# Rows of 520 instead of 512 columns for the x tiles and the h slots of an experts stage

## The chip, the cores and the metric

The kernel runs on one core of one Trainium2 chip, as one program. The metric is the device time of that core in microseconds (us), from the program's start to its end. Lower is better.

## The reference, cut to what matters

The first part is a gated linear attention with a recurrent state. Its output goes through a bilinear layer, and the result `x` (3072 tokens by 384) through four experts whose outputs are added with gate weights. The change is in the experts:

```
def _moe2_ref(x, domain_probs, w1, w2):        # x: 3072 x 384, w1: 4 x 384 x 1024, w2: 4 x 1024 x 384
    E = w1.shape[0]
    p = domain_probs / (domain_probs.sum(-1, keepdims=True) + 1e-09)
    out = np.zeros((N, D), dtype=np.float32)
    for e in range(E):
        h = np.maximum(x @ w1[e], 0.0)
        out += p[:, e:e + 1] * (h @ w2[e])
    return out
```

## The kernel before, in words

All work is in float32. Where a product is large, each operand is split into a high part (rounded to the type fp32r) and the low rest, and one product is made of three: high by high, high by low and low by high (`TERMS` is 3). TensorE therefore has three matmuls where the formula has one.

**Stages.** From 0 to about 414 us of the profiled span, TensorE folds two weight matrices (`w3` and `w_out`) into one, then works on the attention (six chunks of 128 steps in each of four batches) and beside it on the bilinear layer: for each batch two tiles of 384 tokens and eight blocks of 128 features, with `up1` (18 matmuls of 384 columns: line 1022, 1023 and 1024 are its three terms) and `down1` (9 of 384 columns, same lines). The visits to the attention ("visit", lines 1031 to 1084) are short bursts of small matmuls between them. The bilinear layer writes x, high and low part apart, to two DRAM tensors.

**The experts**, from about 414 us to the end, are the stage of the change. The work is four experts `e`, three rounds `m` of each, and 16 steps `s` of a round. A round has two tiles of x of `TILE2` = 512 tokens, tile `u = s // 8`; a step takes block `f = s % 8` of 128 features of h:

- `up2_product` (line 1175) makes h of the step: 9 matmuls of 512 columns, with a 128x128 block of the first weight matrix of the expert as the stationary operand and 512 columns of the x tile as the moving one. `k` is the block of 128 rows of x (three), and the terms are in this order: `we_hi` by `x_hi`, `we_hi` by `x_lo`, `we_lo` by `x_hi`. These are called **up** matmuls below.
- ScalarE writes `h_hi` = relu of the PSUM bank (line 601), VectorE then `h_lo` = relu of the bank minus `h_hi` (line 821). Both have two slots, `s % 2`.
- `down2_product` (line 1294) makes the expert's output: 12 matmuls of 384 columns, with 128 columns of `h_hi` or `h_lo` as the stationary operand and 384 columns of the second weight matrix as the moving one (terms: `h_hi` by `we_hi`, `h_hi` by `we_lo`, `h_lo` by `we_hi`). These are called **down** matmuls below. VectorE adds the sums to `total` with the gate (line 1000).

`step2` writes the order of the two by hand: the 12 down matmuls of step s with the 9 up matmuls of step s + 2 set between them, so that the pattern of seven matmuls "down, down, up, down, up, down, up" runs three times in a step:

```
for i in range(SUBS * TERMS):
    down2_product(e, m, s, i)
    if ahead and i % SUBS >= 1:
        up2_product(ahead[0], ahead[2], ups)
        ups += 1
```

Every matmul has a weight load of its own (the engine row PEld): while one matmul streams its moving operand out of SBUF, the stationary operand of the next one is read out of SBUF too. A pair "A, then B" below is matmul A streaming while B's stationary operand is loaded.

**Loads.** SyncE's queue brings each x tile (high and low part, 768 KB each) into one of two slots (`load_x1`) when the tile that was there has been used up, 24 times in all, and the weights of the next expert once an expert.

**Where the tiles lie.** A partition's tensors lie one after another in the order in which `sb(...)` makes them, each rounded up to 32 bytes. Counted modulo 512 bytes of the partition's address: `h_hi` and `h_lo` start at 480, as do all of the expert's weight tensors (`we_hi`, `we_lo`, both slots), the weights of the bilinear layer (`wb_hi`, `wb_lo`, `wp_hi`, `wp_lo`) and their moving operands (`x0`, `g_hi`, `g_lo`). The four x tiles of the experts (`x1_0_hi`, `x1_0_lo`, `x1_1_hi`, `x1_1_lo`) start at 192. Every row of 512 columns is 2048 bytes and every row of 384 columns 1536 bytes, and every 128 columns are 512 bytes, so that all blocks of a tensor lie at the same address modulo 512 as its start. The distance of a pair is the address of the moving operand minus that of the stationary one that is loaded beside it, modulo 512. Before the change it has two values in the experts: 224 for up, then down (and up, then up), and 0 for down, then down, and for down, then up.

Of the kernel before, what the change touches and what calls it, by code (L numbers as in the profile page):

```python
# [24 lines left out]
F32 = mybir.dt.float32  # L25
F32R = mybir.dt.float32r
ALU = mybir.AluOpType
ACT = mybir.ActivationFunctionType
AX = mybir.AxisListType

P = 128
# [12 lines left out]
KT, FT = DM // P, FF // P  # L44
# [9 lines left out]
TILE2 = 512  # L54
TILES2 = TOKENS // TILE2
SUBS = TILE2 // P
STEPS2 = 2 * FT
ROUNDS = TILES2 // 2
WSET = 2 * KT * FF
PIECE = 512  # L60
# [21 lines left out]
BY_TENSOR = STATES - 1  # L82

ATTENTION_COLUMNS = (SLOTS * 3 + 2 + 2 + 2 + 1) * PAIRS * CHUNK + SLOTS * VD + PAIRS * P + PAIRS * D + PAIRS * ODD + 2 * PAIRS
ATTENTION_REST = ATTENTION_COLUMNS - 4 * KT * TILE2
REDO_X0 = 2 * CHUNKS


def gated_attention_experts(nc, akq, v, akq_long, v_columns, w3T, w_out, wsets, probs, out):
    x1_dram = [nc.dram_tensor(f"x1_{part}_spill", [P, KT, TOKENS], F32, kind="Internal").ap() for part in ("hi", "lo")]  # L90
# [3 lines left out]
    with ExitStack() as ctx:  # L94
        def sb(name, shape, dt=F32, where=ctx):
            return where.enter_context(nc.sbuf_tensor(name, shape, dt))

        def sem(name):
            return ctx.enter_context(nc.semaphore(name))

        bank = [ctx.enter_context(nc.psum_tensor(f"bank{i}", [P, 512], F32)) for i in range(5)]
# [8 lines left out]
        gate = sb("gate", [P, TOKENS // P, EXPERTS])  # L110
        gate_sum = sb("gate_sum", [P, TOKENS // P])
        gate_inv = sb("gate_inv", [P, TOKENS // P])
        h_hi = sb("h_hi", [P, 2, TILE2], F32R)
        h_lo = sb("h_lo", [P, 2, TILE2], F32R)
        outside = sb("outside", [PD, BATCH * CHUNKS])
        outside_sum = sb("outside_sum", [1, 1])
        regular = sb("regular", [1, 1], mybir.dt.int32)
# [49 lines left out]
        we_raw, we_hi, we_lo, x1_hi, x1_lo = [None, None], [None, None], [None, None], [None, None], [None, None]  # L167
# [6 lines left out]


        for slot in range(2):
            x1_hi[slot] = sb(f"x1_{slot}_hi", [P, KT, TILE2], F32R)
            x1_lo[slot] = sb(f"x1_{slot}_lo", [P, KT, TILE2], F32R)
        sb("attention_rest", [P, ATTENTION_REST])
        we_hi[1] = sb("we1_hi", [P, WSET], F32R)  # L180
        raw = ExitStack()
# [84 lines left out]
        x1_loaded = [sem(f"x1_loaded{i}") for i in range(2)]  # L266
        up_done = sem("up_done")
        h_hi_ready = sem("h_hi_ready")
        h_lo_ready = sem("h_lo_ready")
# [49 lines left out]
        def _(sp):  # L319
# [47 lines left out]

            def load_x1(n):
                slot, at = n % 2, n % TILES2 * TILE2
                sp.dma_start(x1_hi[slot][:, :, :].bitcast(F32), x1_dram[0][:, :, at:at + TILE2]).then_inc(x1_loaded[slot], 16)  # L370
                sp.dma_start(x1_lo[slot][:, :, :].bitcast(F32), x1_dram[1][:, :, at:at + TILE2]).then_inc(x1_loaded[slot], 16)

            def load_w3(k):
                sp.dma_start(w3_sb[:, k, 0:FOLD_FIRST * P], w3T[:, k, 0:FOLD_FIRST * P]).then_inc(w3_loaded[k], 16)
# [73 lines left out]
            with sp.If(is_regular == 1):  # L448
                load_x1(0)
                load_x1(1)  # L450
# [3 lines left out]
            with sp.If(is_regular == 0):  # L454
                with sp.Fori(0, BATCH) as b:
                    for t in range(TILES1):
                        store_x1(BATCH + b, t, b * SEQ + t * TILE1)
                sp.wait_ge(x1_stored, X1_AHEAD + 32 * TILES1 * 2 * BATCH)
                load_x1(0)
                load_x1(1)  # L460
            sp.sem_inc(x1_final, 1)
            for e in range(EXPERTS):
# [4 lines left out]
                for tile in range(TILES2):  # L467
# [4 lines left out]
                    if e + 1 == EXPERTS:  # L472
                        count = 1 if tile + 1 == TILES2 else SUBS
                        for i in range(0, SUBS, count):
                            sp.wait_ge(added, ADDED_AHEAD + SUBS * n + i + count)
                            at = slice(tile * SUBS + i, tile * SUBS + i + count)
# [71 lines left out]
        def _(act):  # L548
# [49 lines left out]

            def h_high(n, s):
                act.wait_ge(up_done, STEPS2 * n + s + 1)  # L600
                act.activation(h_hi[:, s % 2, :], bank[s % 2][:, :], ACT.Relu).then_inc(h_hi_ready, 1)  # L601

            def bilinear(b, beside=True, last_batch=False):
                for s in range(STEPS1):
# [75 lines left out]
            with act.If(is_regular == 0):  # L680
                with act.Fori(0, BATCH) as b:
# [26 lines left out]
                    g_high(BATCH + b, 0)  # L708
                    bilinear(BATCH + b, beside=False)
                h_high(0, 0)  # L710


            def round_high(e, m, last):
                for s in range(STEPS2):
                    if s + 1 < STEPS2 or not last:
                        h_high(e * ROUNDS + m, s + 1)
                    if e + 1 < EXPERTS and s % FT == 4:
                        act.wait_ge(x1_final, 1)
                        pieces_high(2 + e, 2 * m + s // FT)

            for e in range(EXPERTS):
                last_expert = e == EXPERTS - 1
                with act.Fori(0, ROUNDS - last_expert) as m:
                    round_high(e, m, False)
            round_high(EXPERTS - 1, ROUNDS - 1, True)


        @block.vector
        def _(dve):
# [88 lines left out]

            def h_low(n, s):
                dve.wait_ge(h_hi_ready, STEPS2 * n + s + 1)  # L820
                dve.scalar_tensor_tensor(out=h_lo[:, s % 2, :], in0=bank[s % 2][:, :], scalar=0.0,  # L821
                                         in1=h_hi[:, s % 2, :], op0=ALU.max, op1=ALU.subtract).then_inc(h_lo_ready, 1)

            def piece_low(i):
                at = slice(i * PIECE, (i + 1) * PIECE)
# [26 lines left out]
            def bilinear(b, beside=True, last_batch=False):  # L852
                for s in range(STEPS1):
# [24 lines left out]
                    if last_batch and beside and s == STEPS1 - 1:  # L878
                        with dve.If(flag == 1):
                            h_low(0, 0)  # L880
# [122 lines left out]
            def round_low(e, m, last):  # L1003
                for s in range(STEPS2):
                    if s + 1 < STEPS2 or not last:
                        h_low(e * ROUNDS + m, s + 1)
                    if s % FT == FT - 1:
                        add(e, m, s // FT)
# [3 lines left out]
            for e in range(EXPERTS):  # L1012
                with dve.Fori(0, ROUNDS - (e == EXPERTS - 1)) as m:
                    round_low(e, m, False)
            round_low(EXPERTS - 1, ROUNDS - 1, True)


        @block.tensor
        def _(pe):
            def split_product(dst, left, right, first, last):  # L1020

                pe.matmul(dst, left[0], right[0], start=first, stop=False)  # L1022
                pe.matmul(dst, left[0], right[1], start=False, stop=False)  # L1023
                return pe.matmul(dst, left[1], right[0], start=False, stop=last)  # L1024
# [145 lines left out]
            def up2_product(e, s, i):  # L1170

                u, f = divmod(s, FT)
                k, term = divmod(i, TERMS)
                cols = slice(k * FF + f * P, k * FF + (f + 1) * P)
                mm = pe.matmul(bank[s % 2][:, :], (we_hi if term < 2 else we_lo)[e % 2][:, cols], (x1_lo if term == 1 else x1_hi)[u][:, k, :],  # L1175
                               start=(i == 0), stop=(i == KT * TERMS - 1))
                if i == KT * TERMS - 1:
                    mm.then_inc(up_done, 1)

            def up2(e, m, s):  # L1180
                up2_waits(e, m, s)
                for i in range(KT * TERMS):
                    up2_product(e, s, i)
# [31 lines left out]
            for k in range(FT):  # L1215
# [5 lines left out]
                for f in range(FOLD_FIRST):  # L1221
                    if (k, f) == (0, 1):
                        pe.wait_ge(w3_loaded[0], 16)
                    cols = slice(f * P, (f + 1) * P)
                    if k < SPLIT_FROM:
                        mm = pe.matmul(bank[FOLD_BANKS[f]][:, 0:DM], w3_sb[:, k, cols], wo_sb[:, k, :], start=(k == 0), stop=False)  # L1226
                    else:
                        i = k - SPLIT_FROM
                        mm = split_product(bank[FOLD_BANKS[f]][:, 0:DM], (w3_hi[:, i, cols], w3_lo[:, k, cols]),
                                           (wo_hi[:, i, :], wo_lo[:, i, :]), False, k == FT - 1)  # L1230
# [7 lines left out]
            for n in range((FT - FOLD_FIRST) * FT):  # L1238
                f, k = FOLD_FIRST + n // FT, n % FT
# [4 lines left out]
                mm = pe.matmul(bank[FOLD_BANKS[f]][:, 0:DM], w3_sb[:, k, f * P:(f + 1) * P], wo_sb[:, k, :], start=(k == 0), stop=(k == FT - 1))  # L1244
# [14 lines left out]
            with nc.body("redo_products", valid_engines=[pe.engine]):  # L1259
                with pe.Fori(0, BATCH) as b:  # L1260
                    with pe.Fori(0, REDO_ROWS) as i:
                        pe.wait_ge(redo_product_ready, REDO_ROWS * b + i + 1)
                        for c in range(CHUNKS):
                            mm = pe.matmul(bank[5][:, 2 * c:2 * c + 2], redo_product[:, c * CHUNK:(c + 1) * CHUNK], head_sum[:, :],
                                           start=True, stop=True)
                        mm.then_inc(redo_summed, 1)
                    for c in range(CHUNKS):
# [3 lines left out]
                        for k in range(KT):  # L1271
                            mm = pe.transpose(bank[7][:, k * P:(k + 1) * P], y_sb[:, k * P:(k + 1) * P], identity[:, :])
# [26 lines left out]
            def step2(e, m, s, ahead):  # L1299

                pe.wait_ge(h_lo_ready, STEPS2 * (e * ROUNDS + m) + s + 1)
                if ahead:
                    up2_waits(*ahead)
                ups = 0
# [5 lines that stand above are left out]
# [72 lines left out]
```

## Time and profile before

| | |
|---|---|
| runs | 1219.95 us median of 3 (1218.94 to 1220.34) |
| profiled execution, span of its instructions | 1217.6 us |
| TensorE busy (matmul) | 1212.3 us, 100% of the span, 7740 matmuls |
| TensorE weight loads busy | 1118.6 us, 92%, 7740 loads |
| VectorE / ScalarE / GpSimd busy | 461.4 / 281.7 / 168.8 us |
| granted TensorE clock | 1.000 of full speed |
| DMA | 108.03 MB, mean 89 GB/s |

The profile is of one execution, whose instructions span 1217.6 us; what lies around the span makes up the rest to the measured time. The busy time of a matmul in it overlaps the next one's (matmuls are pipelined, their ends are modelled), so the time that a matmul takes from the engine is read from the distance between two starts in the timeline, not from its busy time. The timeline prints starts to 0.01 us; over ten or more matmuls that is better than 1 ns each.

### The profile page before, as it was taken

To read this page: it belongs to the slowest core of one execution; us is meant where nothing else is said; L and a number is where in the kernel's file an instruction comes from. 1 tells how busy PE (TensorE), PEld (TensorE's weight loads), DVE (VectorE), ACT (ScalarE), POOL (GpSimd) and SP (SyncE) were. 2 spreads that over 40 slices of the span, in tenths; PEclk is the share of its full clock that TensorE was granted. 3 is DMA by queue.
4 is the path that set the end of the run, shared out by engine and by line. 5 is a ranking of instruction groups with operands and counts; after the bars stand their busy time and mean duration, and the time that the engine had idled before them with its cause. 6 is when DMAs were issued, how large, how long until landed. Compare 5 with 4: busy or idle time off the path is not lost.

```text
span 1217.6 us, 18865 instructions
## 1 busy us (share of the span) xinstructions
PE 1212.3 (100%) x7740; PEld 1118.6 (92%) x7740; DVE 461.4 (38%) x886; ACT 281.7 (23%) x526; POOL 168.8 (14%) x148
## 2 busy tenths in 40 slices
PE   9999999999999999999999999999999999999998
PEld 8799999999999999999999999999999999999998
DVE  6997586586651122122222222222122222222222
ACT  3443333333333311111111111111111111111111
POOL 1132222222223520000000000000000000000000
PEclk9999999999999999999999999999999999999999
DMA  9644444544415331100141111123101111222201
GB/s 286 207 121 122 126 132 106 137 128 105 126 47 195 106 145 52 51 17 36 53 156 52 52 52 52 52 73 135 42 15 46 52 52 53 78 78 78 78 9 44
DMA packets 87543, 108.03 MB, mean 89 GB/s; under 512 B 38576, under 2 KB 57904, under 8 KB 86960
## 3 DMA queue, kind: packets, MB, share of 16 engines
q1 hardware_dynamic: 87184, 106.63, 28.0%
q8 instruction: 52, 0.85, 0.3%
q10 hardware_dynamic: 288, 0.39, 0.1%
q14 instruction: 19, 0.16, 0.0%
HBM read 86.29 MB, written 18.35 MB: 86 GB/s over the span
## 4 chain that ended last, share of the span: by engine, by line
PE 99%; DVE 0%; issue 0%; DVEq 0%; ACT 0%
PE bank L1175 33%; PE bank L1294 25%; PE bank L1022 9%; PE bank L1024 9%; PE bank L1023 9%; PE score_banks L1294 8%; PE bank L1063 2%; PE bank L1244 1%; PE score_banks L1084 1%; PE bank L1073 1%; PE score_banks L1047 1%; PE bank L1226 1%; PE bank L1214 0%; DVE total L1000 0%; PE bank L1031 0%
## 5 line engine op out<-in xcount | busy, mean ns | idle before, releaser
L821 DVE SCALAR_TENSOR_TENSOR h_lo<-bank,h_hi 128x512 fp32r<-128x512 f32 x192 | 132.8, 691 | 584.9 <-ACT h_hi L601 584.0
L601 ACT ACTIVATE h_hi<-bank 128x512 fp32r<-128x512 f32 x192 | 114.7, 597 | 661.7 <-PE bank L1175 661.7
L1175 PE MATMUL bank<-x_hi,we_lo 128*128 128x512 f32 x576 | 228.7, 397 | 0.0
L1175 PE MATMUL bank<-x_hi,we_hi 128*128 128x512 f32 x576 | 224.1, 389 | 0.0
L1175 PE MATMUL bank<-x_lo,we_hi 128*128 128x512 f32 x576 | 223.5, 388 | 0.0
L1294 PE MATMUL bank<-we_hi,h_hi 128*128 128x384 f32 x576 | 194.6, 338 | 0.0
L1294 PE MATMUL bank<-we_lo,h_hi 128*128 128x384 f32 x576 | 194.5, 338 | 0.0
L1294 PE MATMUL bank<-we_hi,h_lo 128*128 128x384 f32 x576 | 193.8, 336 | 0.0
L499 POOL TENSOR_TENSOR we_lo<-we_raw,we_hi (+1 forms) x48 | 60.9, 1289 | 527.8 <-ACT we_hi L562 527.8
L1175 PEld LDWEIGHTS bank<-x_hi,we_lo 128*128 128x128 f32 x576 | 108.3, 188 | 22.4
L1175 PEld LDWEIGHTS bank<-x_lo,we_hi 128*128 128x128 f32 x576 | 108.0, 188 | 22.7
L1022 PE MATMUL bank<-x,wb_hi 128*128 128x384 f32 x384 | 128.6, 335 | 0.0
L1024 PE MATMUL bank<-x,wb_lo 128*128 128x384 f32 x384 | 128.3, 334 | 0.0
L1023 PE MATMUL bank<-x,wb_hi 128*128 128x384 f32 x384 | 128.3, 334 | 0.0
L1294 PEld LDWEIGHTS bank<-we_hi,h_hi 128*128 128x128 f32 x576 | 108.3, 188 | 8.5
L1294 PEld LDWEIGHTS bank<-we_hi,h_lo 128*128 128x128 f32 x576 | 108.3, 188 | 8.4
L1175 PEld LDWEIGHTS bank<-x_hi,we_hi 128*128 128x128 f32 x576 | 108.3, 188 | 0.2
L1294 PEld LDWEIGHTS bank<-we_lo,h_hi 128*128 128x128 f32 x576 | 108.1, 188 | 0.0
L510 POOL TENSOR_TENSOR g_lo<-g_sb,g_hi 128x384 fp32r<-128x384 f32 x64 | 66.3, 1036 | 221.3 <-ACT g_hi L591 221.3
L811 DVE TENSOR_TENSOR g_sb<-a_sb,bank 128x384 f32<-128x384 f32 x64 | 35.3, 552 | 110.8 <-PE bank L1024 110.8
L1022 PEld LDWEIGHTS bank<-x,wb_hi 128*128 128x128 f32 x384 | 72.1, 188 | 0.2 <-issue 0.2
L1023 PEld LDWEIGHTS bank<-x,wb_hi 128*128 128x128 f32 x384 | 72.1, 188 | 0.1
(99 smaller groups left out, 1473.3 us busy)
## 6 DMA issues: line engine op xcount, KB each, us to landing
x_hi<-x_hi_spill SPq DMA_DIRECT2D x24, 768.0 KB, 4.8
x_lo<-x_lo_spill SPq DMA_DIRECT2D x24, 768.0 KB, 6.3
we_raw<-wset SPq DMA_DIRECT2D x4, 3072.0 KB, 10.0
inputs<-akq SPq DMA_DIRECT2D x24, 448.0 KB, 5.2
values<-v_rows SPq DMA_DIRECT2D x24, 256.0 KB, 3.7
inputs<-akq SPq DMA_DIRECT2D x24, 224.0 KB, 3.3
x_hi_spill<-x_hi_out SPq DMA_DIRECT2D x8, 576.0 KB, 4.3
x_lo_spill<-x_lo_out SPq DMA_DIRECT2D x8, 576.0 KB, 5.2
```

The lines of the kernel that those rows point to most:

```text
L499: pool.tensor_tensor(set_lo(n)[:, at], set_raw(n)[:, at], set_hi(n)[:, at], ALU.subtract).then_inc(piece_lo, 1)
L510: pool.tensor_tensor(g_lo[:, s % 2, :], g_sb[:, s % 2, :], g_hi[:, s % 2, :], ALU.subtract).then_inc(g_lo_ready, 1)
L601: act.activation(h_hi[:, s % 2, :], bank[s % 2][:, :], ACT.Relu).then_inc(h_hi_ready, 1)
L811: dve.tensor_tensor(g_sb[:, s % 2, :], a_sb[:, s % 2, :], bank[1][:, 0:TILE1], ALU.mult).then_inc(g_ready, 1)
L821: dve.scalar_tensor_tensor(out=h_lo[:, s % 2, :], in0=bank[s % 2][:, :], scalar=0.0, in1=h_hi[:, s % 2, :], op0=ALU.max, op1=ALU.subtract) ...
L1022: pe.matmul(dst, left[0], right[0], start=first, stop=False)
L1023: pe.matmul(dst, left[0], right[1], start=False, stop=False)
L1024: return pe.matmul(dst, left[1], right[0], start=False, stop=last)
L1047: mm = pe.matmul(bank[5 + half][rows, STATE_AT + i * D:STATE_AT + (i + 1) * D], keys_t[:, pair, rows], values[:, c % SLOTS, at], start=(i ...
L1063: mm = pe.matmul(bank[7][q * ODD:(q + 1) * ODD, (2 * row + g) * CHUNK:(2 * row + g + 1) * CHUNK], values[:, c % SLOTS, at], scores[:, row, ...
L1175: mm = pe.matmul(bank[s % 2][:, :], (we_hi if term < 2 else we_lo)[e % 2][:, cols], (x1_lo if term == 1 else x1_hi)[u][:, k, :], start=(i ...
L1294: mm = pe.matmul(bank[SUM_BANKS[sub]][:, 0:DM], (h_hi if term < 2 else h_lo)[:, s % 2, rows], (we_lo if term == 1 else we_hi)[e % 2][:, cols],
```

## The change

Each row of an x tile and each slot of h becomes 520 columns (2080 bytes) long, of which the first 512 are used as before. `h_rest` and a smaller `attention_rest` fill up, so that what lies behind keeps its address modulo 512 bytes. The number of instructions of every engine, their order, their sizes and their waits stay as they were.

```diff
+SHIFT = 8
...
-ATTENTION_REST = ATTENTION_COLUMNS - 4 * KT * TILE2
+ATTENTION_REST = ATTENTION_COLUMNS - 4 * KT * (TILE2 + SHIFT)
...
-        h_hi = sb("h_hi", [P, 2, TILE2], F32R)
-        h_lo = sb("h_lo", [P, 2, TILE2], F32R)
+        h_hi = sb("h_hi", [P, 2, TILE2 + SHIFT], F32R)
+        h_lo = sb("h_lo", [P, 2, TILE2 + SHIFT], F32R)
+        sb("h_rest", [P, P - 4 * SHIFT])
...
-            x1_hi[slot] = sb(f"x1_{slot}_hi", [P, KT, TILE2], F32R)
-            x1_lo[slot] = sb(f"x1_{slot}_lo", [P, KT, TILE2], F32R)
+            x1_hi[slot] = sb(f"x1_{slot}_hi", [P, KT, TILE2 + SHIFT], F32R)
+            x1_lo[slot] = sb(f"x1_{slot}_lo", [P, KT, TILE2 + SHIFT], F32R)
...
-                sp.dma_start(x1_hi[slot][:, :, :].bitcast(F32), x1_dram[0][:, :, at:at + TILE2]).then_inc(x1_loaded[slot], 16)
+                sp.dma_start(x1_hi[slot][:, :, 0:TILE2].bitcast(F32), x1_dram[0][:, :, at:at + TILE2]).then_inc(x1_loaded[slot], 16)
...
-                act.activation(h_hi[:, s % 2, :], bank[s % 2][:, :], ACT.Relu).then_inc(h_hi_ready, 1)
+                act.activation(h_hi[:, s % 2, 0:TILE2], bank[s % 2][:, :], ACT.Relu).then_inc(h_hi_ready, 1)
...
-                mm = pe.matmul(bank[s % 2][:, :], (we_hi if term < 2 else we_lo)[e % 2][:, cols], (x1_lo if term == 1 else x1_hi)[u][:, k, :],
+                mm = pe.matmul(bank[s % 2][:, :], (we_hi if term < 2 else we_lo)[e % 2][:, cols], (x1_lo if term == 1 else x1_hi)[u][:, k, 0:TILE2],
```

(The load of `x1_lo` and VectorE's `h_lo` change in the same way.)

Modulo 512 bytes the tiles now start at: `x1_0_hi` 192, `x1_0_lo` 288, `x1_1_hi` 384, `x1_1_lo` 480, each with 32 more for `k` = 1 and 64 more for `k` = 2; `h_hi` 480 and 0 in its two slots, `h_lo` 32 and 64. The weights stay at 480. The distances of the pairs become:

| pair | in a step | before | after |
|---|---|---|---|
| up, then down | 9 | 224 | 14 multiples of 32 from 0 to 480 (0 in 144 of 1711 pairs, 224 in 94) |
| down, then down | 3 | 0 | 0 in 197 of 593 pairs, 480 in 198, 448 in 99, 416 in 99 |
| down, then up | 9 | 0 | 0 |

## Rows read from the trace of the kernel before

**Rows 1.** The page: busy share of TensorE, and the granted clock in 40 slices.
```profile
PE 1212.3 (100%) x7740; PEld 1118.6 (92%) x7740; DVE 461.4 (38%) x886; ACT 281.7 (23%) x526; POOL 168.8 (14%) x148
...
PEclk9999999999999999999999999999999999999999
```
**Rows 2.** The page: the chain that ended last, by engine.
```profile
PE 99%; DVE 0%; issue 0%; DVEq 0%; ACT 0%
```
**Rows 3.** Waits in total: who for whom, us, times, longest.
```profile
ACT h_hi L601 <- PE bank L1175: 661.7, 192, 3.8
```
**Rows 4.** The page, DMA issues: count, KB each, us to landing.
```profile
x_hi<-x_hi_spill SPq DMA_DIRECT2D x24, 768.0 KB, 4.8
x_lo<-x_lo_spill SPq DMA_DIRECT2D x24, 768.0 KB, 6.3
```
**Rows 5.** Timeline of PE, bilinear stage, a long run of 384 columns: start, us.
```profile
124.50 0.33 PE L1022 MATMUL bank<-x,wb_hi 128*128 128x384 f32 x1
...
132.12 0.34 PE L1024 MATMUL bank<-x,wb_lo 128*128 128x384 f32 x1
```
**Rows 6.** The same just before, the first matmuls behind a visit to the attention.
```profile
123.08 0.34 PE L1023 MATMUL bank<-g_lo,wp_hi 128*128 128x384 f32 x1
...
123.98 0.33 PE L1022 MATMUL bank<-g_hi,wp_hi 128*128 128x384 f32 x1
```
**Rows 7.** Timeline of PE, last down matmuls of the kernel, without ups between them.
```profile
1210.48 0.34 PE L1294 MATMUL score_banks<-we_hi,h_lo 128*128 128x384 f32 x1
...
1211.38 0.33 PE L1294 MATMUL bank<-we_lo,h_hi 128*128 128x384 f32 x1
1211.55 0.33 PE L1294 MATMUL bank<-we_hi,h_lo 128*128 128x384 f32 x1
...
1214.15 0.34 PE L1294 MATMUL bank<-we_hi,h_lo 128*128 128x384 f32 x1
```
**Rows 8.** Timeline of PE, nine ups in a row, and the first down matmul.
```profile
413.76 0.39 PE L1175 MATMUL bank<-x_hi,we_hi 128*128 128x512 f32 x1
413.98 0.39 PE L1175 MATMUL bank<-x_lo,we_hi 128*128 128x512 f32 x1
...
415.85 0.34 PE L1022 MATMUL bank<-g_hi,wp_hi 128*128 128x384 f32 x1
...
419.62 0.45 PE L1294 MATMUL score_banks<-we_hi,h_hi 128*128 128x384 f32 x1
```
**Rows 9.** Timeline of PE in the experts, one pattern of seven and the next start.
```profile
704.00 0.34 PE L1294 MATMUL bank<-we_lo,h_hi 128*128 128x384 f32 x1
704.17 0.34 PE L1294 MATMUL bank<-we_hi,h_lo 128*128 128x384 f32 x1
704.35 0.39 PE L1175 MATMUL bank<-x_hi,we_hi 128*128 128x512 f32 x1
704.58 0.34 PE L1294 MATMUL bank<-we_hi,h_hi 128*128 128x384 f32 x1
704.75 0.39 PE L1175 MATMUL bank<-x_lo,we_hi 128*128 128x512 f32 x1
704.98 0.34 PE L1294 MATMUL bank<-we_lo,h_hi 128*128 128x384 f32 x1
705.15 0.40 PE L1175 MATMUL bank<-x_hi,we_lo 128*128 128x512 f32 x1
705.39 0.34 PE L1294 MATMUL bank<-we_hi,h_lo 128*128 128x384 f32 x1
```
**Rows 10.** Windows: stretch, us, busy (x count) of PE, PEld, others; PEclk, DMA share, GB/s.
```profile
722.00:1022.00 300.00, 300.00 (x1516) 273.43 (x1515) 71.19 (x108) 52.37 (x90) 22.84 (x18) 1.00 0.17 58
1022.00:1202.00 180.00, 180.00 (x911) 164.04 (x910) 41.52 (x63) 25.68 (x43) 0.00 (x0) 1.00 0.16 57
```
**Rows 11.** The same first stretch, up matmuls alone, then down matmuls alone.
```profile
722.00:1022.00 300.00, 253.88 (x650) 121.90 (x649) 1.00 0.17 58
...
722.00:1022.00 300.00, 257.00 (x866) 162.72 (x866) 1.00 0.17 58
```

More of the change, by code:

```diff
@@ L369, in load_x1 @@
                 slot, at = n % 2, n % TILES2 * TILE2
-                sp.dma_start(x1_hi[slot][:, :, :].bitcast(F32), x1_dram[0][:, :, at:at + TILE2]).then_inc(x1_loaded[slot], 16)
-                sp.dma_start(x1_lo[slot][:, :, :].bitcast(F32), x1_dram[1][:, :, at:at + TILE2]).then_inc(x1_loaded[slot], 16)
+                sp.dma_start(x1_hi[slot][:, :, 0:TILE2].bitcast(F32), x1_dram[0][:, :, at:at + TILE2]).then_inc(x1_loaded[slot], 16)
+                sp.dma_start(x1_lo[slot][:, :, 0:TILE2].bitcast(F32), x1_dram[1][:, :, at:at + TILE2]).then_inc(x1_loaded[slot], 16)
             def load_w3(k):
@@ L820, in h_low @@
                 dve.wait_ge(h_hi_ready, STEPS2 * n + s + 1)
-                dve.scalar_tensor_tensor(out=h_lo[:, s % 2, :], in0=bank[s % 2][:, :], scalar=0.0,
-                                         in1=h_hi[:, s % 2, :], op0=ALU.max, op1=ALU.subtract).then_inc(h_lo_ready, 1)
+                dve.scalar_tensor_tensor(out=h_lo[:, s % 2, 0:TILE2], in0=bank[s % 2][:, :], scalar=0.0,
+                                         in1=h_hi[:, s % 2, 0:TILE2], op0=ALU.max, op1=ALU.subtract).then_inc(h_lo_ready, 1)
             def piece_low(i):
```

## The prediction

> **What bounds the kernel now.** I read the page first: TensorE is busy for the whole span, at the full granted clock in every slice [rows 1], and the chain that ended last is 99% TensorE [rows 2]. No other engine is in it: in the experts ScalarE waits for the up matmuls 192 times, 661.7 us in all [rows 3]. So only a change in the distance from one matmul's start to the next one's moves the time, and the rest of the reading is of those distances, in the timeline.
>
> The full clock is the 2.4 GHz level. At one column a cycle 384 columns are 160.0 ns and 512 columns are 213.3 ns. In a long run of 384 columns in the bilinear stage there are 44 distances from 124.50 to 132.12 us, 7.62 us, so 173.2 ns each [rows 5]; at the kernel's end 15 down matmuls take 2.60 us, 173.3 ns each [rows 7]. The plain cost of a matmul is thus its stream and 13.3 ns more. All these pairs are at distance 0 (moving and loaded operand at the same address modulo 512).
>
> Two places show that it can be more. Behind a visit the first 5 distances of a run take 0.90 us, 180 ns each [rows 6], and so do 5 of the first when the ups end (1210.48 to 1211.38) [rows 7]; then the run falls back to 173.3. And the 9 ups in a row ahead of the experts, all at distance 224, take 2.09 us [rows 8]: 232.2 ns each where stream and 13.3 would be 226.7, and these do not settle.
>
> The experts mix both. One pattern of four downs and three ups takes 1.39 us [rows 9]; four times 173.3 and three times 226.7 are 1.373. The long window gives it better: 300 us hold 1516 matmuls [rows 10], 650 of them up and 866 down [rows 11], and 650 x 226.67 + 866 x 173.33 ns are 297.44 us. So 2.56 us of each 300, or 0.85%, are **excess** over the plain cost. The mixed part begins with the first down at 419.62 [rows 8] and ends where the last downs run alone, at 1210.48 [rows 7]; it is 790.9 us long, and its excess is 790.9 x 2.56 / 300 = 6.8 us. It does not come from other traffic: with a DMA share of 0.16 instead of 0.17 the matmuls follow at 911 / 180 = 5.06 per us, against 5.05 [rows 10].
>
> **The change part by part.** It adds no instruction, moves none, and changes no size of an operand.
>
> *ScalarE and VectorE.* Their h accesses stay 512 columns in a row. A cost of 0; even if one got slower, ScalarE sits idle for 3.8 us at the longest before each h [rows 3], and the h of a step is wanted two steps of some 4.16 us later (300 us / 1516 x 21).
>
> *The loads of x.* Each partition now gets three pieces of 2048 bytes at a step of 2080 bytes where it got them end to end. The source was three pieces before. They land in 4.8 and 6.3 us [rows 4], and a tile is used for 8 steps, 33 us, before its slot is wanted again; the other slot covers that time. Twice the landing time would still be hidden, so the cost is 0. Without that cover it would be 24 tiles of some 6 us, 150 us.
>
> *The matmul pairs.* This is the only part on the path. In a step of 21 pairs, the 9 down-then-up pairs keep distance 0. The 9 up-then-down pairs go from 224 to a spread of values, and the 3 down-then-down pairs go from 0 to something else two times in three. There are about 190 such steps.
> - The lower bound of the cost is that all the excess was caused by the distance 224, and goes: -6.8 us, the whole of it.
> - The upper bound is that each of the 12 changed pairs costs what a disturbed pair costs behind a visit, 180 - 173.3 = 6.7 ns: 12 x 6.7 ns x 190 = +15.3 us, with none of the present excess given back.
> - I take 0. The same extra of 13.3 ns is in the plain runs whatever the operands are, and the disturbed distances behind a visit are at distance 0 [rows 6]: an excess of this size is there without any distance, and it comes where the rhythm of the matmuls is broken. A mix of 384 and 512 columns breaks it in every pattern. That is the nearest row for the excess of the experts, and no distance is needed to explain it.
>
> The rows behind a visit [rows 6] show that two streams out of SBUF disturb each other or that a queue refills; they do not tell which. The Trainium skill says on this in "SBUF — State Buffer", section "Who interferes with whom", that TensorE has two independent read ports, one for the moving operand and one for weight loads, and that it never waits for anyone; by that rule the change is worth exactly 0. No run here shows the ports, and the 232.2 ns of the ups in a row [rows 8] speak a little against it. Another rule speaks for more than the excess being at stake: "TensorE: Matmul & The Clock Gate", section "Back-to-back issue gap", gives N/2.4 + 2.5 ns for a matmul, and an estimate by it for a step (9 x 215.8 + 12 x 162.5) is 3.89 us where the trace has 4.16; the trace disagrees with it for this kernel by 0.26 us a step.
>
> **The sum** is 0. Against the profiled execution it leaves the span at 1217.6 us, with 2.35 us around it to the median of the runs, so the forecast is that median, 1219.95, or 1220.0 us.
>
> **The rivals.**
>
> *A. The spread disturbs more (slower).* Place: the 12 changed pairs of every step. Two of the three down-then-down pairs leave distance 0, the only distance at which a run has been seen to settle, and cost 6.7 ns each, 13.4 ns; the 9 up-then-down pairs, whose patterns now carry (2.56 us / 300 us) x 4.16 us = 36 ns a step, rise by some 2.5 ns each, from 4.0 (36 ns over 9 pairs) towards 6.7, another 24 ns. Together 37 ns x 190 = 7.1 us: 1227.1 us. It decides as soon as a new distance costs more than 224 does, on average over the spread. For it: the runs at distance 0 settle, the one at 224 does not, and a rhythm that differs from pair to pair finds no place to settle. Against: the mixed stage never settles as it is.
>
> *B. The distance 224 was a bad one (faster).* Place: the 9 up-then-down pairs. Only 94 of 1711 remain at 224, and if that distance alone made the excess, 0.95 x 6.8 = 6.4 us go: 1213.5 us. For it: the ups in a row never settle [rows 8], and the up with `we_lo` (705.15 to 705.39, 0.24 us) is longer than the one with `we_hi` (704.35 to 704.58, 0.23) in a stage where all else is alike [rows 9]. Against: these two ups have the same x tile and the same distance, so the distance modulo 512 is not what tells them apart; and the ups in a row are also the only run of 512 columns, so that their 232.2 ns may be the size's and not the distance's.
>
> *C. The 13.3 ns themselves hang on the addresses (much faster).* If 12 of 21 pairs lost the whole of it, 12 x 13.3 x 190 = 30.3 us would go: 1189.6 us. Against it: it is the same at distance 0 with 384 columns and, within 6 ns, at 224 with 512.
>
> *D. The change does not do what it says.* The addresses follow from the sizes in the code, so the distances do change; but if only distances above 512 bytes mattered, it would be as without an effect, and this is counted with the forecast.
>
> **How the numbers follow.** A measurement of this kernel can tell about 0.2%, or 2.4 us, from no change. No effect, or one within 2.4 us: 0.42. Rival A with more than 2.4 us: 0.32. Rival B with more than 2.4 us, at any size up to 6.8: 0.24. Rival C: 0.02. So faster is 0.26, same 0.42 and slower 0.32. The likeliest case gives the time, 1220.0. Its own range is 1217.5 to 1222.5. For 8 in 10 the range takes in most of B, to its full price at about 1213, and of A beyond its price of 1227.1, to 1229, two thirds of the way to its bound at 1235.
>
> **What would show it.** In the changed kernel's timeline the run in the bilinear stage [rows 5] should stay at 173.2 ns. The last downs [rows 7] show whether pairs that are 32 to 96 bytes away from 0 still settle: 15 of them in 2.60 us if distances don't matter, in 2.70 if each costs 6.7 ns. The nine ups in a row [rows 8] should take 2.09 us; 2.04 would speak for B. The count of matmuls in a 300 us window should be 1516 by the forecast [rows 10], 1528 by B, 1503 by A. The DMA rows should land as before. The prediction is wrong if that count moves by more than 3; its failing step would be the 0 that I took for the matmul pairs.

## The result and the profile after

| | before | after |
|---|---|---|
| median of 4 runs each | 1219.45 us (1218.33 to 1220.34) | 1225.06 us (1224.10 to 1225.63) |
| span of the profiled execution | 1217.6 us | 1223.7 us |
| first down matmul to last down matmul | 794.5 us (419.62 to 1214.15) | 800.2 us (420.03 to 1220.25) |

The ratio is 1.0046, with a 95% interval of 1.0031 to 1.0060: slower by 5.6 us. That is inside the wide range of the prediction and is its rival A; the forecast of the likeliest case, no change, was wrong, and its own range (1217.5 to 1222.5) was left.

The page of the kernel after says the same as before of who bounds it [rows 1, 4]: TensorE at 100%, the granted clock full, the loads of x as quick as they were.

```profile
span 1223.7 us, 18865 instructions
PE 1218.1 (100%) x7740; PEld 1117.4 (91%) x7740; DVE 461.7 (38%) x886; ACT 282.6 (23%) x526; POOL 168.9 (14%) x148
...
PEclk9999999999999999999999999999999999999999
...
x_hi<-x_hi_spill SPq DMA_DIRECT2D x24, 768.0 KB, 4.8
x_lo<-x_lo_spill SPq DMA_DIRECT2D x24, 768.0 KB, 6.4
```

The windows of the kernel after (columns as in [rows 10]) have the loss: the same 300 us hold 1505 matmuls instead of 1516, with an unchanged DMA share.

```profile
722.00:1022.00 300.00, 300.00 (x1505) 271.13 (x1505) 70.51 (x107) 52.51 (x90) 22.88 (x18) 1.00 0.17 58
1022.00:1202.00 180.00, 180.00 (x904) 162.69 (x903) 42.91 (x66) 25.78 (x43) 0.00 (x0) 1.00 0.16 57
```

The timeline of its PE tells where. The long run in the bilinear stage, none of whose operands changed places modulo 512, has its 44 distances in 7.62 us as before [rows 5]. Here are the nine ups in a row ahead of the experts, then the first down, then the last 16 downs of the kernel:

```profile
414.16 0.39 PE L1177 MATMUL bank<-x_hi,we_hi 128*128 128x512 f32 x1
...
416.24 0.33 PE L1024 MATMUL bank<-g_hi,wp_hi 128*128 128x384 f32 x1
...
420.03 0.44 PE L1296 MATMUL score_banks<-we_hi,h_hi 128*128 128x384 f32 x1
...
1217.62 0.34 PE L1296 MATMUL bank<-we_hi,h_lo 128*128 128x384 f32 x1
...
1220.25 0.34 PE L1296 MATMUL bank<-we_hi,h_lo 128*128 128x384 f32 x1
```

The ups in a row take 2.08 us where they took 2.09 [rows 8]: 0.01 us less. The 15 distances of the last downs take 2.63 us where they took 2.60 [rows 7]: 175.3 ns each instead of 173.3. So neither of the two pure runs has much of the loss. It is in the mix. Taken over every start of the mixed part (the trace holds them to 1 ns), and counted over the plain 226.7 or 173.3 ns:

| pair | in a step | before, ns over plain | after | change in a step |
|---|---|---|---|---|
| up, then down | 9 | 1.7 | 5.7 | +36.6 |
| down, then up | 9 | 2.5 | 1.5 | -9.2 |
| down, then down | 3 | 0.8 | 1.7 | +2.6 |
| sum of a step | 21 | 40 | 70 | +30 |

30 ns in each of some 190 steps are 5.7 us, which is the whole difference of the two stretches above (800.2 - 794.5).

Below, the **excess** of a step is its time over 21 plain matmuls (9 x 226.67 + 12 x 173.33 ns = 4.120 us): 40 ns before, 70 after. One tile slot serves 8 steps in a row, so a kernel can hold two layouts, one for each slot, and its trace shows each by itself.

### The profile page after: what moved, and what is told of

Its sections match the earlier page's. It is cut to its first block, busy times and chain, and to the rows that moved or that the text cites. A ratio compares the mean times of both kernels' runs of the same rounds, so it can differ in the third digit from the quotient of the medians.

```text
span 1223.7 us, 18865 instructions
## 1 busy us (share of the span) xinstructions
PE 1218.1 (100%) x7740; PEld 1117.4 (91%) x7740; DVE 461.7 (38%) x886; ACT 282.6 (23%) x526; POOL 168.9 (14%) x148
## 4 chain that ended last, share of the span: by engine, by line
PE 98%; DMA 1%; DVE 1%; SPq 0%; ACT 0%; issue 0%; DVEq 0%; ACTq 0%
PE bank L1177 33%; PE bank L1296 25%; PE bank L1024 9%; PE bank L1026 9%; PE bank L1025 9%; PE score_banks L1296 8%; PE bank L1065 2%; PE bank L1246 1%; PE score_banks L1086 1%; PE bank L1075 1%; PE score_banks L1049 1%; DMA wo_sb<-w_out 1%; DVE total L1002 0%; PE bank L1033 0%; DVE w_lo L898 0%; DVE suffix L742 0%
## 5 line engine op out<-in xcount | busy, mean ns | idle before, releaser
L1177 PE MATMUL bank<-x_lo,we_hi 128*128 128x512 f32 x576 | 227.2, 394 | 0.0
L1177 PE MATMUL bank<-x_hi,we_hi 128*128 128x512 f32 x576 | 226.6, 393 | 0.0
```

## The experiments

### x520 and h520: each half of the change alone

`x520` makes only the rows of the x tiles 520 columns long, `h520` only the slots of h.

```diff
 x520:
+SHIFT = 8
...
+            x1_hi[slot] = sb(f"x1_{slot}_hi", [P, KT, TILE2 + SHIFT], F32R)
+            x1_lo[slot] = sb(f"x1_{slot}_lo", [P, KT, TILE2 + SHIFT], F32R)
...
 h520:
+SHIFT = 8
...
+        h_hi = sb("h_hi", [P, 2, TILE2 + SHIFT], F32R)
+        h_lo = sb("h_lo", [P, 2, TILE2 + SHIFT], F32R)
+        sb("h_rest", [P, P - 4 * SHIFT])
...
```

> Rows of 520 columns for the x tiles alone; h as before, so the down-then-down pairs stay at distance 0 and the up-then-down pairs are at 192 to 480 and 0 (from -288 in steps of 32). Theory P (the distance of a pair, moving operand minus the stationary one loaded beside it, modulo 512, sets what the pair costs): the trace after the change has the up-then-down pairs at 5.7 ns over their plain 226.7 against 1.7 before, so this alone gives most of the loss, 1223.5 to 1225.5 us. Rival S (what costs is only that the distances differ from pair to pair and the rhythm never settles; both halves of the change do that alike): half of the loss, about 1222 us. Rival N (down-then-down pairs away from 0 are what costs): 1219.5 us.

> Slots of 520 columns for h alone; x tiles as before. Up-then-down pairs are at 224, 192, 160 and 128, down-then-down pairs at 0, 480, 448 and 416. Theory P: by the means of the trace after the change at those distances (6.3, 7.6, 3.4, -0.9 ns) the up-then-down pairs rise from 1.7 to some 4 ns and the down-then-down pairs by 1 to 3 ns; 1220.5 to 1224 us. Rival S: about 1222 us. Rival N: the whole loss, 1225 us. Rival W (only moving operands off a multiple of 512 bytes cost, weight loads do not care): 1219.5 us.

Measured: `x520` 1222.86 us, ratio 1.0038 (1.0024 to 1.0051) to 1219.07 before; `h520` 1219.72 us, ratio 1.0007 (0.9998 to 1.0016). Their windows:

```profile
722.00:1022.00 300.00, 300.00 (x1508) 271.79 (x1507) 70.42 (x107) 52.35 (x90) 22.86 (x18) 1.00 0.17 58
```
```profile
722.00:1022.00 300.00, 300.00 (x1515) 272.71 (x1514) 71.19 (x108) 52.62 (x90) 22.86 (x18) 1.00 0.17 58
```

The x rows alone bring 3.8 of the 5.6 us, the h slots 0.7. The interval of `h520` includes 0, but its steps don't: from the first down matmul to the last, `x520` takes 4.0 us more than the kernel before and `h520` 0.65, where the change takes 5.7, so together the halves bring 1.0 us more than their sum. `x520` is a little under what theory P gave, and `h520`, with 43 to 45 ns a step, is under its range of 1220.5 to 1224: the prices at a distance read from the trace after the change don't carry over to another kernel. The same distance has another price in another mix. Rival W of `h520` (only the places of moving operands cost) gave 1219.5 us, which its time fits; it falls below, where `h_lo_32` moves nothing but an operand of weight loads and every step changes. Rival S (only that the distances differ from pair to pair) and rival N (the down-then-down pairs) have both fallen: in `h520` the distances differ from pair to pair and down-then-down pairs are away from 0, and it costs next to nothing.

### all_shifted: distances kept, every address moved

```diff
+        sb("h_ahead", [P, 24])
         h_hi = sb("h_hi", [P, 2, TILE2], F32R)
```

> The kernel before with 96 bytes ahead of h, so that h, the x tiles and all weights and everything behind them move by 96 bytes and every distance stays. Theory P: nothing changes, 1219.5 us, and up-then-down 1.7, down-then-up 2.5, down-then-down 0.8 ns over plain as before. Rival A (the address of an operand itself modulo 512, not its distance to the other, is what costs): another time, 2 to 8 us away.

Measured: 1218.72 us, ratio 1.0000 (0.9991 to 1.0009). In the window there are 1516 matmuls, as before [rows 10], and every step has its 40 ns of excess. So the operands' addresses by themselves cost nothing (96 bytes is the one shift that was tried), and what the change cost comes from their differences.

```profile
722.00:1022.00 300.00, 300.00 (x1516) 273.44 (x1516) 71.19 (x108) 52.37 (x90) 22.83 (x18) 1.00 0.17 58
```

### Constant distances of x, two in each kernel

Rows of 512 columns everywhere; only where the tiles of slot 0 and of slot 1 begin is moved, by columns that nothing uses (`X_PADS` is (72, 32) for `x_d0_d128`, and so on).

```diff
+X_PADS = (72, 32)
...
+ATTENTION_REST = ATTENTION_COLUMNS - 4 * KT * TILE2 - sum(X_PADS)
...
         for slot in range(2):
+            if X_PADS[slot]:
+                sb(f"x_pad{slot}", [P, X_PADS[slot]])
```

> Rows of 512 columns everywhere, but the x tiles of slot 0 start at 480 (distance 0 to h and to the weights, in steps 0 to 7 of each round) and those of slot 1 at 96 (distance 128, in steps 8 to 15). No distance differs from pair to pair within a tile. Theory P: both halves settle on a period of their own, clearly different from each other and from 4.157 us a step at 224; distance 0 is expected to lose the excess (4.12 us a step) as the long runs at 0 do, distance 128 too, since the up-then-down pairs at 128 in the trace after the change are 0.9 ns under the plain cost; in all 1212 to 1214 us. Rival S: any constant distance is as good as 224, 1219.5 us and equal steps in both halves.

> Constant distances again, 64 in the first half of each round (tile slot 0), 96 in the second (slot 1). So far a step of 21 matmuls at a constant distance has cost over its plain 4.120 us: 40 ns at 224, 121 at 0, 57 to 84 at 128. Theory P1 (a pair is dear while the two streams are in the same place, and the cost falls smoothly with the distance): between 121 and 57, so 80 to 110 ns. Rival P2 (the cost jumps with the distance, since it hangs on when the rhythm of seven matmuls meets the same place): no order, anywhere from 0 to 120.

> Constant distances 160 (slot 0) and 192 (slot 1). P1: falling from 57 to 84 ns at 128 to 40 at 224, so 45 to 75 ns a step. P2: no order. Whether one of them is under the 40 ns of 224, and so faster than the kernel before, is open in both.

> Constant distances 256 (slot 0) and 288 (slot 1), just on the other side of 224. P1: 256 is as far from 0 as can be, so it has the minimum, 40 ns or less a step, and 288 much the same: 1217 to 1219.5 us. P2: no order.

> Constant distances 352 (slot 0) and 416 (slot 1), the near side of 0 from below. P1, if the cost is symmetric about 0: like 160 and 96, 50 to 110 ns a step. P1 with a direction (the moving stream runs faster than the weight load, so a start just behind it catches up and one just ahead runs away): these would differ clearly from 160 and 96. P2: no order.

Measured: `x_d0_d128` 1229.46 us, ratio 1.0087 (1.0073 to 1.0100), the slowest of all where the fastest was expected. The others, in the order above, are one measurement each, beside 1218.88 for the kernel before on the same chip: 1224.63, 1224.73, 1227.83 and 1226.78 us. The excess comes from the timeline of PE, by the start of the first down matmul of a step and of the same one six steps later. (The ups run two steps ahead, so the last two of a slot's eight steps already stream the other slot's tile and are left out.) The kernel before, `x_d0_d128` (distance 0) and `x_d256_d288` (distance 256), all in the first half of round 1 of expert 1:

```profile
685.97 0.34 PE L1294 MATMUL score_banks<-we_hi,h_hi 128*128 128x384 f32 x1
...
710.93 0.34 PE L1294 MATMUL score_banks<-we_hi,h_hi 128*128 128x384 f32 x1
```
```profile
689.38 0.34 PE L1297 MATMUL score_banks<-we_hi,h_hi 128*128 128x384 f32 x1
...
714.82 0.34 PE L1297 MATMUL score_banks<-we_hi,h_hi 128*128 128x384 f32 x1
```
```profile
688.90 0.34 PE L1297 MATMUL score_banks<-we_hi,h_hi 128*128 128x384 f32 x1
...
714.34 0.34 PE L1297 MATMUL score_banks<-we_hi,h_hi 128*128 128x384 f32 x1
```

Six steps are 24.96, 25.44 and 25.44 us, so 4.160, 4.240 and 4.240 a step, 40, 120 and 120 ns over plain. The same for 96 (`x_d64_d96`, second half of the same round) and 352 (`x_d352_d416`, first half), then for 160 (`x_d160_d192`, first half) and 416 (`x_d352_d416`, second half):

```profile
716.39 0.34 PE L1297 MATMUL score_banks<-we_hi,h_hi 128*128 128x384 f32 x1
...
741.59 0.34 PE L1297 MATMUL score_banks<-we_hi,h_hi 128*128 128x384 f32 x1
```
```profile
688.40 0.34 PE L1297 MATMUL score_banks<-we_hi,h_hi 128*128 128x384 f32 x1
...
713.60 0.34 PE L1297 MATMUL score_banks<-we_hi,h_hi 128*128 128x384 f32 x1
```
```profile
687.64 0.34 PE L1297 MATMUL score_banks<-we_hi,h_hi 128*128 128x384 f32 x1
...
712.84 0.34 PE L1297 MATMUL score_banks<-we_hi,h_hi 128*128 128x384 f32 x1
```
```profile
717.79 0.34 PE L1297 MATMUL score_banks<-we_hi,h_hi 128*128 128x384 f32 x1
...
742.99 0.34 PE L1297 MATMUL score_banks<-we_hi,h_hi 128*128 128x384 f32 x1
```

All four are 25.20 us, 4.200 a step, 80 ns. In this way:

| distance of x | excess of a step, ns | the same distance plus 256 |
|---|---|---|
| 0 | 120 | 256: 120 |
| 32 | not tried | 288: 50 |
| 64 | 60 | |
| 96 | 80 | 352: 80 |
| 128 | 57 and 84, in turns | |
| 160 | 80 | 416: 80 |
| 192 | 60 | |
| 224 (before) | 40 | |

Three things follow. First, the distance has a price, and it is far from small at its worst: 80 ns a step from 224 to 0. Second, in all three pairs that were tried the cost **repeats after 256 bytes**, and not only in the sum: in `x_d0_d128` and `x_d256_d288` the starts follow each other with the same pattern to within 2 ns, as they do for 96 and 352, and for 160 and 416 if one of them is shifted by one pattern of seven. The 512 of the change's title is one period too many. Third, it is no smooth fall with the distance from 0 (P1 expected the minimum at 128 or 256) and not without order either (P2). Counted from the nearest multiple of 256, 0 is the worst place and the places 32 beside it are the best (224 at 40, 288 at 50); from there the cost rises with the distance, 60 and 60 at 64 on either side, 80 and 80 at 96, and 57 to 84 at 128. So 256, the worst, lies right between the two best, and the kernel before happened to sit on the best of the eleven. The sums agree with the times: for `x_d0_d128` ((120 + 70) / 2 - 40) ns x 190 = 10.5 us, measured 10.4; for `x_d256_d288` ((120 + 50) / 2 - 40) x 190 = 8.6, measured 9.0.

The change itself goes through fourteen such distances, and its 70 ns a step is what the average over the eight places within 256 bytes is in the table (with 288 for 32 and the middle of 57 and 84). That it lost because it left the best one for an average one fits this, but is not shown: the two halves of the change don't add up, and a price can't be given to a single pair.

### h_moved: distance to what?

In all of these h and the weights lay at the same place. Here h moves alone (and the weights of every other expert with it).

```diff
+        sb("h_ahead", [P, 56])
         h_hi = sb("h_hi", [P, 2, TILE2], F32R)
         h_lo = sb("h_lo", [P, 2, TILE2], F32R)
+        sb("h_behind", [P, 72])
...
+X_PADS = (0, 72)
...
+        sb("we1_ahead", [P, 32])
         we_hi[1] = sb("we1_hi", [P, WSET], F32R)
```

> So far the cost of a step over 4.120 us repeats with 256 bytes: 120 ns at a distance of 0 and 256, 80 at 96, 160, 352 and 416, 60 at 64 and 192, 40 to 50 at 224 and 288. In all of these h and the weights lay at the same place, so the distance may be to either. Here both h parts start at 192 (224 bytes further than before), the x tiles of slot 0 at 192 and those of slot 1 at 480, the weights of experts 0 and 2 at 480 and those of experts 1 and 3 at 96. Rule H (moving x against the loaded h, which is how I counted the distance): distance 0 in the first half of each round, 120 ns a step, and 288 in the second, 50 ns, in all experts alike. Rule W (moving x against the weights, that is against the moving operand of the down matmuls around it and the operand loaded for the next up): experts 0 and 2 have 224 in the first half, 40 ns, and 0 in the second, 120 ns; experts 1 and 3 have 96 in the first half, 80 ns, and 128 in the second, 57 to 84 ns. If all distances count together, including weights against h (288 and 96 here, 0 before), neither row of numbers comes out.

Measured: 1223.42 us (before: 1219.23, one measurement each). The excess of a step, from the first down matmul of a step and of the one six later, in expert 2 and then in expert 1, the first half of round 1 in both:

```profile
887.64 0.34 PE L1300 MATMUL score_banks<-we_hi,h_hi 128*128 128x384 f32 x1
...
912.84 0.34 PE L1300 MATMUL score_banks<-we_hi,h_hi 128*128 128x384 f32 x1
```
```profile
686.57 0.34 PE L1300 MATMUL score_banks<-we_hi,h_hi 128*128 128x384 f32 x1
...
711.61 0.34 PE L1300 MATMUL score_banks<-we_hi,h_hi 128*128 128x384 f32 x1
```

They are 25.20 and 25.04 us, so 80 and 53 ns over plain for each step.

| experts, slot | x to h | x to weights | h to weights | rule H | rule W | measured |
|---|---|---|---|---|---|---|
| 0 and 2, slot 0 | 0 | 224 | 224 | 120 | 40 | 80 |
| 0 and 2, slot 1 | 288 | 0 | 224 | 50 | 120 | 60 |
| 1 and 3, slot 0 | 0 | 96 | 96 | 120 | 80 | 53 |
| 1 and 3, slot 1 | 288 | 384 | 96 | 50 | 57 to 84 | 80 |

(Distances modulo 512, the first operand minus the second. For the last row the expectation writes 128; the addresses give 384, which has no measurement of its own and is priced like 128 by the repeat after 256.) Neither rule comes out, as the expectation's last sentence had it for the case that all distances count. With x 224 from the weights, moving h doubled the excess; with x right on h, it was 80 or 53 and not 120. "The distance of a pair", which the prediction and theory P counted, is therefore too simple: what the mix costs hangs on where all three kinds of operand lie to each other.

### parts_we_lo and parts_h_lo: a search over the low parts

Four layouts in each, two by tile slot and two by expert. `parts_we_lo` puts the low weights 128 bytes (experts 0, 2) or 32 bytes (1, 3) behind the high ones; `parts_h_lo` puts the low h part 32 bytes behind the high one, and all weights of experts 1 and 3 by 32. In both, one of the two x slots has its high and low tile 64 bytes apart modulo 256 (224 and 32).

```diff
 parts_we_lo:
+X_PADS = ((0, 0), (0, 80))
...
+        sb("we0_between", [P, 32], F32, first)
...
+        sb("we1_between", [P, 8])
...
 parts_h_lo:
+X_PADS = ((0, 0), (80, 48))
...
         h_hi = sb("h_hi", [P, 2, TILE2], F32R)
+        sb("h_between", [P, 8])
         h_lo = sb("h_lo", [P, 2, TILE2], F32R)
+        sb("h_behind", [P, 120])
...
+        sb("we1_ahead", [P, 8])
...
```

> A search for a layout better than the one before, four in one kernel, and at once a question: does the low part of the weights have a distance of its own. The low weights lie 128 bytes further than the high ones for experts 0 and 2, and 32 further for experts 1 and 3; the x tiles of slot 0 are both at 224, those of slot 1 at 224 (high) and 32 (low). Theory Q (all three distances count: x to h, x to weights, weights to h; the cost of a step comes in lots of 20 ns, that is of 6.7 ns for each pattern of seven matmuls): each of the four settles on a step of its own, at 20 to 100 ns over 4.120 us, and every pattern of seven costs the same unless x high and low differ. A layout under 40 ns, if there is one among them, beats the kernel before. Rival: the low weights don't matter, and slot 0 stays at 40 in all four experts.

> Four more: the low h part 32 bytes further than the high one; x tiles of slot 0 both at 224, of slot 1 at 32 (high) and 224 (low) from the h of before; the weights of experts 1 and 3 moved by 32 bytes. Theory Q: each of the four has a step of its own, 20 to 100 ns over 4.120 us. With h alone on a spread (h520) a step was 43 to 45 ns, so experts 0 and 2 in slot 0 are expected at 40 to 50. Rival: a step is at 40 wherever x is 224 from the high h, so slot 0 in all experts.

Measured (one measurement each, before 1219.76): 1223.87 and 1223.76 us. `parts_we_lo` has 60 ns in slot 0 for both kinds of experts, and in slot 1 67 for experts 0 and 2, 58 and 62 in turns for 1 and 3, so the low weights do have a distance of their own: 128 or 32 bytes off cost 20 ns against the 40 of before. `parts_h_lo` has 87 ns in experts 1 and 3 in both slots, where all weights moved by 32 bytes; 40 in experts 0 and 2, slot 1; and in their slot 0, where nothing but the low h part has moved, 26.7. That is well below the 40 to 50 expected there from `h520`: again a price did not carry over from one layout to another. In these layouts the excess is close to a multiple of 6.7 ns, which is 16 cycles of the full clock, and at the constant distances it is mostly 40, 60, 80 or 120. Exceptions are those at 128 and 288, the 58 and 62 ns here, and the 43 ns of `h520`; and the multiple is one of the step, not always of each pattern of seven (at 160 and 416 the three patterns have 25, 31 and 25 ns).

### h_lo_32: the best of them as a kernel

```diff
         h_hi = sb("h_hi", [P, 2, TILE2], F32R)
+        sb("h_between", [P, 8])
         h_lo = sb("h_lo", [P, 2, TILE2], F32R)
+        sb("h_behind", [P, 120])
```

> The kernel before with the low h part alone 32 bytes further, which is what experts 0 and 2 had in the first half of each round of parts_h_lo, at 26.7 ns a step over 4.120 us instead of 40. Theory Q: all 190 steps take 26.7, so 13.3 ns x 190 = 2.5 us less than before: about 1216.6 us, ratio 0.998, and 1521 matmuls in the window from 722 to 1022 us. Rival (the 26.7 hung on its neighbours in that kernel, the other experts and tiles): steps not all at 26.7, and 1219 us.

Measured: 1216.42 us, ratio 0.9977 (0.9968 to 0.9986) to 1218.97 before: 2.5 us faster, as expected to 0.2 us. All steps of all experts have 26.7 ns. Its window, and six steps of its first half of round 1 of expert 1 in the timeline of PE (24.88 us, 4.147 a step):

```profile
722.00:1022.00 300.00, 300.00 (x1521) 273.83 (x1520) 71.90 (x109) 52.94 (x91) 22.83 (x18) 1.00 0.17 58
```
```profile
684.47 0.34 PE L1296 MATMUL score_banks<-we_hi,h_hi 128*128 128x384 f32 x1
...
709.35 0.34 PE L1296 MATMUL score_banks<-we_hi,h_hi 128*128 128x384 f32 x1
```

It beats both the kernel before and the change, by two tensors that nothing reads or writes.

The last downs of the kernel show something more, as no ups are between them. First the 15 last distances here, then those of `h_moved`:

```profile
1208.36 0.34 PE L1296 MATMUL bank<-we_hi,h_lo 128*128 128x384 f32 x1
...
1211.00 0.34 PE L1296 MATMUL bank<-we_hi,h_lo 128*128 128x384 f32 x1
```
```profile
1215.64 0.34 PE L1300 MATMUL bank<-we_hi,h_lo 128*128 128x384 f32 x1
...
1218.24 0.34 PE L1300 MATMUL bank<-we_hi,h_lo 128*128 128x384 f32 x1
```

They are 2.64 us, 176.1 ns each by the starts to 1 ns, and 2.60 us, 173.3 ns each. The window of the first has no ScalarE, no GpSimd and no DMA beside TensorE and four adds of VectorE:

```profile
1208.35:1210.95 2.60, 2.60 (x16) 2.60 (x16) 1.20 (x4) 0.00 (x0) 0.00 (x0) 1.00 0.00 0
```

In `h_moved` every down here has its moving operand 96 bytes from the loaded one and pays nothing; in `parts_we_lo` the moving operand itself is in two places by turns, and the mean is 173.2. Only where the stationary operands lie in more than one place (`h_lo_32`, `parts_h_lo`, `h520` and the change) does this run take 175.1 to 176.5 ns. So in a pure run it is not the distance that the prediction counted, moving against stationary, that costs.

## Why the prediction was right or wrong

- **What bounds the kernel**: right. All that changed is the distance between matmul starts, and only in the experts.
- **The order, ScalarE, VectorE and the loads of x at 0**: right. Landing is 4.8 and 6.4 us [rows 4], and the counts of instructions are the same.
- **The measure of the plain cost and of the excess**: right in the main, and it carried the rest. 0.85% over plain is 36 ns a step by the window and 40 by the single starts, and each later kernel's time followed from its excess to half a us. The one exception is `h_moved`: its steps give +5.4 us, and its experts do take 5.2 us more, but in that one execution the part ahead of them took 1.2 us less than in the trace of the kernel before, so that the whole was 4.2 slower. Two readings were a little off. The window gave 36 ns where the single starts give 40, because the count of a window takes in the matmuls that lie across its ends (300 / 4.160 x 21 is 1514, not 1516); the excess of the kernel before is thus 40 ns x 190 = 7.6 us and not 6.8. And the disturbed pairs behind a visit are 178.6 ns each by the starts to 1 ns, so 5.3 ns over plain and not 6.7.
- **The 0 for the matmul pairs**: this is the step that failed. The prediction took it since "an excess of this size is there without any distance, and it comes where the rhythm of the matmuls is broken". The first half of that is true (rows behind a visit are at distance 0 [rows 6]), but it does not follow that the distance adds nothing: the same broken rhythm costs 40 ns a step at one distance and 120 at another. Measured: +30 ns a step where 0 was taken, and by the prediction's own sign (a count of matmuls more than 3 away from 1516) the count of 1505 refutes it. That the measured time is inside the stated range is owed to the width that was given to the rivals, not to this term.
- **Rival A (slower, 0.32)**: this is what happened, with 7.1 us forecast and 5.6 measured, 1503 matmuls in the window forecast and 1505 measured. Its terms were less good than its sum. Up-then-down was to rise by 2.5 ns and rose by 4.1; down-then-down was to cost 13.4 ns a step and cost 2.6; down-then-up was left at 0 change and gave back 9.2. That the sum came so near is in part luck. Its ground was wrong too: it held that distance 0 is the good one, as runs settle there, and in the mix a constant 0 is the worst that was found. The last downs show 175.3 ns where A's price would have given 180.
- **Rival B (224 was a bad distance, 0.24)**: the opposite is so. It is the best of the eleven constant distances that were run. The nine ups in a row, which spoke for B [rows 8], take the same 2.1 us after the change, and 2.07 to 2.10 us in every layout that was run, so at least 3.1 of their 5.6 ns over plain are not the distance's. Whether the size of 512 columns or the order makes it is open.
- **Rival C (the 13.3 ns)**: nothing of it was seen in any kernel.
- **Rival D (it does not do what it says)**: fell with the pairs; in what was tried, a distance of x counts only modulo 256 bytes.
- **The Trainium skill on ports**: "SBUF — State Buffer", section "Who interferes with whom", of the Trainium skill has TensorE with two independent read ports and waiting for nobody, and the prediction read a worth of exactly 0 out of it. The traces disagree with that 0: with equal instructions the same step takes 4.147 to 4.240 us by nothing but where its operands lie.
- **The lower bound**: -6.8 us for all excess gone (7.6 by the steps). It was not passed; the best layout found gets 2.5 us of it.

What stays open: by what part of the chip the operands meet. That the weight load and the moving stream disturb each other in SBUF fits the runs, since differences of addresses count and the addresses don't, and since three kinds of operand are in play. But there is a rival that no run rules out: one weight load against the next, and one moving stream against the next. The last downs speak for a part of it, as there only stationary operands in different places cost. No run separates the two reads from each other, and the price in lots of 6.7 ns and the period of 256 bytes are measured, not explained. Starts finer than 32 bytes, x high against x low by themselves, and layouts of all five tensors at once were not tried, so 26.7 ns is the best found and not the least there is.

## What to carry to other kernels

When TensorE is the bound and its matmuls are already back to back, take the distance between two starts from the timeline, subtract the stream (columns at the granted clock) and the constant that the cleanest run shows (here 13.3 ns). What is left is a cost of layout or rhythm that can be measured to a nanosecond. Here it moved a kernel by -0.2 to +0.9% with the same instructions in the same order, so a pad ahead of a tensor is a change that has to be timed, and any other edit that happens to move a tensor can bring such a difference with it. A trace can test several layouts at once, one for each buffer slot and stage; take the best as a kernel of its own, and don't carry a price from one mix of matmuls over to another.

## What had not been expected of the hardware

- A step of 21 matmuls takes 4.147 to 4.240 us by its operands' relative places alone; moving all of them by 96 bytes together changes nothing (1.0000).
- The effect of the x tile's place repeats after 256 bytes: 120 and 120 ns at 0 and 256, 80 and 80 at 96 and 352, 80 and 80 at 160 and 416. The worst place (0) is 32 bytes from the best (224, 40 ns, and 288, 50 ns).
- The two pure runs show little of it: over all kernels here the last 15 downs take 173.2 to 176.5 ns each, over 173.3 only where the slots or the two parts of h lie apart and not where the weights lie 96 bytes from h, and the nine ups 2.07 to 2.10 us. The mix shows 93 ns a step between the best and the worst layout.
- The excess of a step is close to a multiple of 6.7 ns in most layouts.
